# Recurrence and feed-forward block on one core: the first batch's spans cut as 488, 4 x 512, 504 pairs instead of 480, 5 x 512

## What is computed

```python
sig = 1.0 / (1.0 + np.exp(-f_logit))
f = lower_bound + (1.0 - lower_bound) * sig
for t in range(S):
    h = f[:, t] * h + (1.0 - f[:, t]) * x[:, t]
    y[:, t] = h
# feed-forward, rows are the tokens of y
h = y @ w_in
g = np.where(h >= 1, h, np.where(h <= -1, 0.0, (h + 1) ** 2 / 4))
out = g @ w_out
```

## Time and profile before

| what | value |
|---|---|
| time, median of 3 runs | 993.77 us |
| time of the profiled execution | 994.05 us |
| its span, first to last instruction | 992.0 us |
| TensorE busy | 986.2 us, 99% |
| TensorE weight load busy | 817.7 us, 82% |
| ScalarE busy | 873.0 us, 88% |
| VectorE busy | 865.5 us, 87% |
| DMA, mean | 43 GB/s |
| granted TensorE clock | 1.00 |

### The profile page before, as it was taken

One profiled execution on the slowest core, in us unless ns is written; L12 is line 12 of the kernel. 1 busy time (PEld: TensorE's weight loads), 2 busy tenths in 40 slices (PEclk: granted clock), 3 DMA queues, 4 the chain that ended last, 5 costly groups with the idle time before them and its releaser, 6 DMA issues.

```text
span 992.0 us, 12870 instructions
## 1 busy us (share of the span) xinstructions
PE 986.2 (99%) x4366; PEld 817.7 (82%) x4366; DVE 865.5 (87%) x1305; ACT 873.0 (88%) x1543; POOL 0.2 (0%) x4
## 2 busy tenths in 40 slices
PE   9999999999999999999999999999999999999998
PEld 6888888888888888888888888888888888888887
DVE  7998988988888988898888989889898889898775
ACT  8898889989988988998998898899898899898886
POOL 0000000000000000000000000000000000000000
PEclk9999999999999999999999999999999999999999
DMA  6202102101200210210120020021021012000101
GB/s 233 101 1 86 41 1 85 44 1 43 86 1 1 85 43 1 85 43 1 44 85 1 23 82 24 1 83 43 1 79 50 0 42 83 1 1 1 43 1 41
DMA packets 14577, 42.37 MB, mean 43 GB/s; under 512 B 1584, under 2 KB 4912, under 8 KB 14512
## 3 DMA queue, kind: packets, MB, share of 16 engines
q1 hardware_dynamic: 14368, 41.56, 12.3%
q10 hardware_dynamic: 144, 0.00, 0.0%
HBM read 29.10 MB, written 12.45 MB: 42 GB/s over the span
## 4 chain that ended last, share of the span: by engine, by line
PE 97%; ACT 1%; DVE 0%; issue 0%; ACTq 0%; DVEq 0%
PE acc L914 17%; PE acc L915 17%; PE acc L916 17%; PE chain L914 8%; PE chain L915 8%; PE chain L916 8%; PE cross L915 4%; PE cross L914 4%; PE cross L916 4%; PE side L914 2%; PE side L915 2%; PE side L916 2%; PE side L1116 1%; ACT g L370 0%; PE side L1072 0%
## 5 line engine op out<-in xcount | busy, mean ns | idle before, releaser
L914 PE MATMUL acc<-g_hi,w_out_lo 128*128 128x512 f32 (+2 forms) x768 | 297.6, 387 | 0.0
L916 PE MATMUL acc<-g_hi,w_out_hi 128*128 128x512 f32 (+2 forms) x768 | 297.3, 387 | 0.0
L915 PE MATMUL acc<-g_lo,w_out_hi 128*128 128x512 f32 (+2 forms) x768 | 297.3, 387 | 0.0
L730 DVE TENSOR_TENSOR g_lo<-g,g_hi 128x512 fp32r<-128x512 f32 (+2 forms) x384 | 261.6, 681 | 8.5 <-ACT g_hi L395 0.5
L395 ACT CAST g_hi<-g 128x512 fp32r<-128x512 f32 (+2 forms) x384 | 235.3, 613 | 38.2 <-DVE g L715 32.5
L388 ACT ACTIVATE g<-g 128x512 f32<-128x512 f32 (+2 forms) x384 | 240.7, 627 | 3.9
L715 DVE SCALAR_TENSOR_TENSOR g<-g,h 128x512 f32<-128x512 f32 (+1 forms) x264 | 180.8, 685 | 46.1 <-ACT g L388 43.0
L370 ACT ACTIVATE g<-h 128x512 f32<-128x512 f32 (+1 forms) x264 | 162.8, 630 | 27.4 <-DVE h L690 24.8
L914 PEld LDWEIGHTS acc<-g_hi,w_out_lo 128*128 128x128 f32 x768 | 144.1, 188 | 29.7 <-DVE g_lo L730 1.0
L916 PEld LDWEIGHTS acc<-g_hi,w_out_hi 128*128 128x128 f32 x768 | 144.1, 188 | 28.5
L915 PEld LDWEIGHTS acc<-g_lo,w_out_hi 128*128 128x128 f32 x768 | 144.1, 188 | 28.3
(11 more groups left out here) (83 smaller groups left out, 952.8 us busy)
## 6 DMA issues: line engine op xcount, KB each, us to landing
gate<-f_logit_chunks SPq DMA_DIRECT2D x18, 512.0 KB, 3.8
y<-x_chunks SPq DMA_DIRECT2D x18, 512.0 KB, 4.1
out_chunks<-result SPq DMA_DIRECT2D x9, 1024.0 KB, 4.2
w_out_f<-w_out_pairs SPq DMA_DIRECT2D x8, 256.0 KB, 4.7
y<-x_chunks SPq DMA_DIRECT2D x4, 496.0 KB, 4.0
gate<-f_logit_chunks SPq DMA_DIRECT2D x4, 496.0 KB, 3.9
w_in_near<-w_in_pairs SPq DMA_DIRECT2D x10, 128.0 KB, 4.5
out_chunks<-result SPq DMA_DIRECT2D x1, 992.0 KB, 4.2
```

Source lines behind the costliest of these rows:

```text
L730: nc.vector.tensor_tensor(g_lo[:, t, 0:cols], g[:, t, 0:cols], g_hi[:, t, 0:cols].bitcast(f32), ALU.subtract).then_inc(g_lo_ready[t], 1)
L914: nc.tensor.matmul(dst, w_lo, v_hi, start=start, stop=False, skip_group_check=more)
L915: nc.tensor.matmul(dst, w_hi, v_lo, start=False, stop=False, skip_group_check=more)
L916: return nc.tensor.matmul(dst, w_hi, v_hi, start=False, stop=stop, skip_group_check=more)
```

## The change

`width(q)` gives 488 for span 0 instead of 480, and 504 for span 10 instead of 512. Both are spans of the first batch, which keeps its 3040 pairs: 488 + 4 x 512 + 504 = 480 + 5 x 512. Spans 2, 4, 6 and 8 keep 512 pairs but start 16 tokens later. The second batch (496, 4 x 512, 496) is untouched. No instruction is added, removed or moved on any engine; those of spans 0 and 10 (and what prepares and stores these spans) have other sizes, and the raw products of span 0 go in halves of 244.

```diff
 SPANS = 12
-FULL, FIRST_SHORT, LAST_SHORT = 512, 480, 496
+FULL = 512
+
+SHORT = {0: 488, SPANS - 2: 504, SPANS - 1 - BATCH: 496, SPANS - 1: 496}
...
 def width(q):
-    if q == 0:
-        return FIRST_SHORT
-    return LAST_SHORT if q in (SPANS - 1 - BATCH, SPANS - 1) else FULL
+    return SHORT.get(q, FULL)
```

## The result

| | kernel before | changed kernel |
|---|---|---|
| time, median of 10 runs | 993.81 us | 996.47 us |
| lowest to highest | 993.36 to 994.44 | 996.08 to 996.90 |
| profiled execution | 994.05 us | 996.08 us |
| its span | 992.0 us | 994.1 us |

The ratio is 1.0027, 95% interval 1.0019 to 1.0035: 2.7 us slower. The forecast was 992.9 us with a range to 994.5 and 4% for anything slower by over 0.2%. It was wrong in size and in sign.

The account below looks back on a forecast made before the run. TensorE, busy 986.2 of 992.0 us, was taken as the bound. Terms 0 - 1.20 + 0.34 + 0.02 - 0.10 = -0.94 us gave a median of 992.8, stated as 992.9 us, range 992.0 to 994.5.

Parts of the forecast that it names:

- the price of a column: TensorE matmuls: width + 32 cycles, with a floor near 520 cycles read as the weight load.
- its three prices: Distances between matmul starts read from the profile: 216.6 ns at 480 columns, 220.0 at 496, 226.7 at 512.
- Span 10, -1.20 us: TensorE in span 10: 360 matmuls go from 544 to 536 cycles at 504 columns, -1.20 us.
- My rival of steps: Widths charged in steps of 16 columns: span 10 gains nothing, span 0 pays 1.20 us; 995.2 us, 7%.
- Span 0 on TensorE, 0: 360 matmuls of span 0 at 488 columns stay at 520 cycles, as at 480: 0 us.
- My upper bound of 1.20: Span 0 on TensorE: 8 cycles more for each of 360 matmuls if the price is linear, 1.20 us.
- a rival of 13%: Linear at 488: width + 40, so 488 takes 528 cycles and span 0 pays 1.20 us; 994.0 us, 13%.
- The opening and VectorE, +0.34: Span 0: wider loads and VectorE instructions make TensorE leave the handover of 40.77 us 0.34 us later.
- 0.17 us: Opening: wider loads and VectorE work delay the first split product from 15.69 to 15.86 us.
- VectorE's unbroken row: Span 0 from 23.08 us: 14 VectorE instructions, 9 ns longer each, add 0.13 us before a low part.
- The wait in span 9, -0.10: `p4` at 808.01 us: a narrower cast ahead of its copy may remove the wait and its wake, -0.10 us.
- The third and fourth rivals: Third: waits for ScalarE's copies in span 10's windows, 996.2 us, 3%. Fourth: slower opening loads, 994.8 us, 6%.

Follow-up runs that it names:

- run 8: Not a label of a run: the words belong to "can run 8 cycles below that line", said of 496 columns at 528 cycles and 512 at 544.
- experiment 1: Kernel without the computation: rows of 60 matmuls at 464 to 512 columns, some with a hold-up; 488 columns in fp32r measured 541 cycles, 528 after a hold-up.
- experiment 2: Kernel without the computation: rows of 40 matmuls, each behind one of another width; seven of nine 488 rows ran at 540 to 547 cycles.
- experiment 7: Span 1's drive and channel group 1's forget gate moved later: 996.60 us on the changed kernel, 995.78 with spans 0 and 10 at 496, 993.36 on the kernel before.
- experiments 4 to 6: Widths of spans 0 and 10 set to 496 and 496 (995.06 us), 488 and 496 (994.99), 496 and 496 with span 1's drive moved (995.56).
- experiment 6: Span 1's drive moved behind a low part: 996.58 us on the changed kernel, 995.56 on its second kernel (spans 0 and 10 at 496), 993.55 on the kernel before.

## Why the prediction was wrong

**The failed step is the price of a column.** "Width + 32 gives 520 cycles for 488, just the floor that 480 pays already: 0." There is no such floor near 520 (464 columns take 504), and the line is not width + 32 but width + 40, so that 488 pays 528 at best; in span 0 it mostly paid 541.5. The two rows from which I drew the slope, 496 at 528 and 512 at 544, are the two widths that can run 8 cycles below that line; 480 was the ordinary one. Three widths gave me a bend, and I explained the wrong one of them as the exception. Behind that stood a cause that nothing had tested: the weight load's recorded 187 ns is shorter than any distance here, and experiment 1 has it at 187 ns in the row of 464 columns too, which stand 210 ns apart. With the floor falls the prediction's sentence that its three prices, as they are not on one line, speak for weight load and matmul together. What the 40 cycles consist of is open.

**Span 10, -1.20 us: measured 0.** By width + 40, 504 takes 544 cycles, what 512 takes. My rival of steps gave the same number for another reason. The prediction took the term as lying "on the slope that the rows show"; that slope was the one between the two exceptions.

**Span 0 on TensorE, 0: measured +2.6 us on its matmuls, hold-ups in it.** My upper bound of 1.20, 8 cycles a matmul, holds for the cheap way (528) and not for the way that 488 takes most of the time (about 541). Nothing in the profile of before showed a width running at 20 cycles over another 8 columns narrower. What it did show is that one width can have two prices: the 496 wide matmuls behind 808.01. I used that for a rival of 13% and gave it the smaller price.

**The opening and VectorE, +0.34: measured -0.59 in the opening and no growth behind it.** The first split product came earlier, at 15.10. VectorE's second drive began at 6.32 instead of 7.00:

```profile
6.32 0.70 DVE L592 SCALAR_TENSOR_TENSOR y<-gate,one_minus_lb,y 128x488 f32<-128x488 f32 x1
```

It did not wait for a DMA there: the load landed at 6.17 us, before the change at 6.91. Over all profiles the first split product starts at 15.6 to 15.8 with 480 (four), at 15.1, 15.2, 15.3 and 15.7 with 488, and at 15.6, 15.6, 15.8 and 16.0 with 496. When the loads land varies by more than my whole term, so 0.17 us could not be told from one trace. The arithmetic of VectorE's unbroken row, 14 instructions of 9 ns, was of no account once TensorE became slower than VectorE in span 0: of the later hold-ups none was left. My cost was worked out for a TensorE that keeps its pace.

**The wait in span 9, -0.10: no gain.** It is still there at 809.91, with 0.28 us to the next start instead of 0.33, and the 536 cycles behind it stayed; the stretch to the end is 0.20 longer.

**The rivals.** Width + 40 was in the text as the first, at 13%, but applied to span 0 alone; applied to span 10 as well it would have given 993.8 + 1.5 = 995.3. No case had the 541 cycles that carry the rest. The third and fourth rivals did not occur: no distance over 590 cycles in span 10, and the load that VectorE waited for came earlier. That the third rival's 996.2 lies near the measured time is chance.

**Open.** What decides between the ways, and why the dear way of 488 has a longer distance every seventh matmul, is not settled. The runs show that a row has its way from its first matmuls on (experiment 2), that behind a pause of 1.0 and of 1.9 us 488 ran cheap both times (experiment 1; in one of them it had before), that 480 columns ran 8 cycles dearer where the operand began 8 columns into its tile (1), and that neither hold-ups (7) nor other engines' traffic (1) are needed for the dear way.

## What to carry to other kernels

Take the price of a matmul from its own width in its own type, measured, before trading columns between spans; a slope between two widths says nothing of a third one 8 columns away. Prefer widths that kept one price through all rows and spans (here 504 and 512 in fp32r, and 480 where the operand begins with its tile) to ones with two, even where the second price can be lower: the three kernels with three or four spans of 496 in experiments 4 to 6 spread over 2.3 to 3.5 us, and their medians were 1.3 to 1.7 us above the kernel before, while the best single run of all was 0.9 below its fastest. And put a stretch's length distribution beside its mean: 382/382/383 against 382/386/408 would have shown in one line what no view of waits does.

## What the runs showed of the hardware that I had not expected

- fp32r matmuls of 464 to 504 columns in steps of 8, each with its own weights, are columns + 40 cycles apart at best in experiment 1; 512 takes columns + 32, and 496 took columns + 32 through whole spans of the kernel. 480 columns that begin 8 columns into their tile took columns + 48. bf16 is columns + 6.
- 488 columns have two lasting ways: 528 cycles each, and a cycle of seven distances (in experiment 7 530, 530, 533, 581, 545, 535, 538) with a mean near 541. 496 has 528 and 536.
- The cheap way ended at a single distance 6 to 7 ns too long, at 37.46 us in experiment 6 (488 columns) and at 809.48 us in its second kernel (496).
